# Reordering the attention stage of a retention / MoE kernel: state updates, masks, key scaling and loads

## The reference

```python
gamma = 1.0 - 2.0 ** (-5.0 - np.arange(H, dtype=np.float32))
scale = 1.0 / np.sqrt(D)
state = np.zeros((B, H, D, D), dtype=np.float32)
for t in range(S):
    state = gamma[None, :, None, None] * state + np.einsum('bhd,bhe->bhde', k[:, :, t], v[:, :, t])
    y[:, :, t] = scale * np.einsum('bhd,bhde->bhe', q[:, :, t], state)
```

## Time and profile before

| | us |
|---|---|
| median of 3 runs | 441.89 |
| lowest, highest | 439.13, 443.94 |
| the profiled execution, its own time | 442.01 |
| its span, first to last instruction | 440.3 |
| mean granted TensorE clock | 0.982 of full speed |
| PE busy | 416.1 (95%) |
| DVE, ACT, POOL busy | 211.0 (48%), 196.1 (45%), 154.5 (35%) |

### The profile page before, as it was taken

The page is one execution under the profiler, slowest core; times in us unless marked ns, Lnnn a source line. Parts: engine busy times, 40 slices in busy tenths (PEclk is TensorE's granted clock), DMA queues, the critical chain, the costliest instruction groups (busy, mean ns, idle before and its releaser), DMA issues.

```text
span 440.3 us, 7192 instructions
## 1 busy us (share of the span) xinstructions
PE 416.1 (95%) x2619; PEld 349.8 (79%) x2620; DVE 211.0 (48%) x288; ACT 196.1 (45%) x275; POOL 154.5 (35%) x127
## 2 busy tenths in 40 slices
PE   6699999999999999999659999999999999999992
PEld 3588889897889987878548888888888888888862
DVE  4478838874004878474322612225662261725340
ACT  2234567861214865551612812225771381826440
POOL 3430974000000000025851732213883164563661
PEclk9889999999999999999997999999999999999998
DMA  8979900000420009451573174011288317457100
GB/s 301 416 297 376 423 11 1 0 1 0 155 100 33 1 1 367 205 193 65 222 290 141 49 283 188 30 44 49 69 361 341 118 48 281 151 200 270 35 28 11
DMA packets 15577, 67.75 MB, mean 154 GB/s; under 512 B 2559, under 2 KB 3583, under 8 KB 11200
## 3 DMA queue, kind: packets, MB, share of 16 engines
q1 hardware_dynamic: 12352, 58.88, 34.1%
q0 software_dynamic: 2912, 8.13, 5.6%
q10 hardware_dynamic: 288, 0.41, 0.3%
HBM read 58.49 MB, written 10.22 MB: 156 GB/s over the span
## 4 chain that ended last, share of the span: by engine, by line
PE 86%; DMA 4%; POOL 3%; issue 2%; ACT 1%; SPq 1%; DVE 0%; POOLq 0%; DVEq 0%
PE ps L953 24%; PE ps L955 23%; PE ps L954 23%; PE ps L1240 3%; DMA kv<-qkv 3%; POOL wx L426 3%; PE ps L983 3%; PE ps L1004 2%; PE ps L1001 2%; PE ps L1202 2%; DMA xg<-x_rows,gnow 2%; PE ps L1054 1%; PE ps L967 1%; ACT wx L568 1%; PE ps L1063 1%
## 5 line engine op out<-in xcount | busy, mean ns | idle before, releaser
L426 POOL TENSOR_TENSOR wx<-raw_w,wx 128x1024 fp32r<-128x1024 f32 x21 | 53.5, 2563 | 14.7 <-ACT wx L568 14.6
L953 PE MATMUL ps<-wx,hT 128*128 128x512 f32 x136 | 55.6, 409 | 0.7 <-POOL wx L426 0.7
L568 ACT CAST wx<-raw_w 128x1024 fp32r<-128x1024 f32 x56 | 54.8, 1057 | 1.8 <-issue 1.3
L953 PE MATMUL ps<-wx,xT 128*128 128x512 f32 x136 | 54.6, 402 | 1.0 <-DVE xT L884 0.9
L955 PE MATMUL ps<-wx,hT 128*128 128x512 f32 x136 | 53.8, 396 | 0.0
L954 PE MATMUL ps<-wx,hT 128*128 128x512 f32 x136 | 53.8, 396 | 0.0
L955 PE MATMUL ps<-wx,xT 128*128 128x512 f32 x136 | 53.1, 391 | 0.0
L954 PE MATMUL ps<-wx,xT 128*128 128x512 f32 x136 | 53.0, 390 | 0.0
L628 ACT CAST hT<-ps 128x512 fp32r<-128x512 f32 x34 | 18.3, 591 | 59.5 <-PE ps L1240 59.3
L875 DVE TENSOR_TENSOR wx<-raw_w,wx 128x1024 fp32r<-128x1024 f32 x35 | 42.5, 1262 | 4.6 <-ACT wx L568 3.9
L884 DVE TENSOR_TENSOR xT<-ps,xT 128x512 fp32r<-128x512 f32 x17 | 11.8, 692 | 68.7 <-ACT xT L621 68.7
(11 more groups left out here) (161 smaller groups left out, 809.3 us busy)
## 6 DMA issues: line engine op xcount, KB each, us to landing
raw_w<-w_exp SPq DMA_DIRECT2D x28, 1024.0 KB, 8.0
qk<-qkv SPq DMA_DIRECT2D x7, 768.0 KB, 7.6
kv<-qkv SPq DMA_DIRECT2D x6, 768.0 KB, 9.5
raw_first<-w_exp SPq DMA_DIRECT2D x4, 1024.0 KB, 7.9
x_rows<-x2n SPq DMA_DIRECT2D x12, 256.0 KB, 2.4
x_early<-x2n SPq DMA_DIRECT2D x10, 256.0 KB, 2.1
win_raw<-w_in SPq DMA_DIRECT2D x4, 512.0 KB, 8.9
woutT<-w_out_t SPq DMA_DIRECT2D x1, 2048.0 KB, 13.1
```

Source lines behind the costliest of these rows:

```text
L426: ins = nc.gpsimd.tensor_tensor(wx[:, slot, 1, c], raw, wx[:, slot, 0, c].bitcast(F32), ALU.subtract)
L568: nc.scalar.copy(wx[:, slot, 0, c], raw).then_inc(wx_hi[w], 1)
L953: mm(o, lh, rl, start=first, stop=False)
```

## The change

Four things move, and no arithmetic is added or taken away.
- PE: `updates(i + 1)` stands behind `scores(i + 1, 0)` for every i, not ahead of `values(i, 0)`.
- DVE: `mask(i, 0)` stands ahead of `scan(i)`.
- ACT: `k_scale(i + 2)` stands behind the two copies of pair i.
- SP: `kv` of pairs 2 and 3 comes as keys and values apart (384 KB each), the decay tables of pairs 2 and 3 as 192 KB each behind that pair's values, each with its own semaphore; `updates(i)` waits for the values of pairs 0 to 3, `k_scale` only for the keys.

```diff
--- before.py
+++ after.py
@@ -214,13 +214,14 @@
 
 
         decay0_in = sem("decay0_in")
-        const_in, decay_in, small_in = sem("const_in"), sem("decay_in"), sem("small_in")
+        const_in, small_in = sem("const_in"), sem("small_in")
         first_in, half_in, k0_in = sem("first_in"), sem("half_in"), sem("k0_in")
         loaded = sem("loaded")
         qk_in = [sem(f"qk_in{i}") for i in range(4)]
         kv_in = [sem(f"kv_in{i}") for i in range(4)]
         win_in, wout_in = [sem(f"win_in{n}") for n in range(4)], sem("wout_in")
-        k1_in, decay1_in = sem("k1_in"), sem("decay1_in")
+        k_in = [k0_in] + [sem(f"k_in{i}") for i in range(1, NP_)]
+        decay_in = [decay0_in] + [sem(f"decay_in{p}") for p in range(1, NP_)]
         raw_w1_in = [[sem(f"raw_w1_in{i}{a}") for a in range(2)] for i in range(2)]
         raw_first_in = [[sem(f"raw_first_in{w}{a}") for a in range(2)] for w in range(2)]
         raw_w2_in = [sem(f"raw_w2_in{a}") for a in range(2)]
@@ -324,21 +325,21 @@
             sp.dma_start(kv[0][:, 1, :], qkv[0, :, 3, :]).then_inc(kv_in[0], 16)
             sp.dma_start(decay[:, 0], decay_c[:, 0]).then_inc(decay0_in, 16)
             sp.dma_start(qk[0][:, :, HALF:S], qkv[0, :, 0:2, HALF:S]).then_inc(qk_in[0], 16)
-            sp.dma_start(qk[1][:], qkv[1, :, 0:2, :]).then_inc(qk_in[1], 16)
-            sp.dma_start(kv[1][:, 0, :], qkv[1, :, 2, :]).then_inc(k1_in, 16)
-            sp.dma_start(decay[:, 1], decay_c[:, 1]).then_inc(decay1_in, 16)
-            sp.dma_start(kv[1][:, 1, :], qkv[1, :, 3, :]).then_inc(kv_in[1], 16)
-            for i in range(2, B * NP_):
+            for i in range(1, NP_):
+                sp.dma_start(qk[i][:], qkv[i, :, 0:2, :]).then_inc(qk_in[i], 16)
+                sp.dma_start(kv[i][:, 0, :], qkv[i, :, 2, :]).then_inc(k_in[i], 16)
+                if i == 1:
+                    sp.dma_start(decay[:, i], decay_c[:, i]).then_inc(decay_in[i], 16)
+                sp.dma_start(kv[i][:, 1, :], qkv[i, :, 3, :]).then_inc(kv_in[i], 16)
+                if i > 1:
+                    sp.dma_start(decay[:, i], decay_c[:, i]).then_inc(decay_in[i], 16)
+            for i in range(NP_, B * NP_):
                 j = i % 4
-                if i >= 4:
-                    sp.wait_ge(pv_done, 2 * (i - 4) + 2)
+                sp.wait_ge(pv_done, 2 * (i - 4) + 2)
                 sp.dma_start(qk[j][:], qkv[i, :, 0:2, :]).then_inc(qk_in[j], 16)
-                if i == 2:
-                    sp.dma_start(decay[:, 2:], decay_c[:, 2:]).then_inc(decay_in, 16)
                 sp.dma_start(kv[j][:], qkv[i, :, 2:4, :]).then_inc(kv_in[j], 16)
-                if i >= 4:
-                    c = slice(1024 * (i - 4), 1024 * (i - 4) + 1024)
-                    sp.dma_start(win_raw[:, c], w_in[:, c]).then_inc(win_in[i - 4], 16)
+                c = slice(1024 * (i - 4), 1024 * (i - 4) + 1024)
+                sp.dma_start(win_raw[:, c], w_in[:, c]).then_inc(win_in[i - 4], 16)
                 if i == 5:
                     sp.dma_start(con[:], const_c).then_inc(const_in, 16)
             sp.dma_start(cvw[:], conv_w).then_inc(small_in, 16)
@@ -401,11 +402,8 @@
                 pool.wait_ge(qk_in[j], 16 * (i // 4 + 1))
                 if i == 0:
                     pool.wait_ge(half_in, 16)
-                    pool.wait_ge(decay0_in, 16)
-                if i == 1:
-                    pool.wait_ge(decay1_in, 16)
-                if i == 2:
-                    pool.wait_ge(decay_in, 16)
+                if i < NP_:
+                    pool.wait_ge(decay_in[i], 16)
                 qd = decay[:, p, 2, :].unsqueeze(1).to_broadcast([P, CH, P])
                 nc.gpsimd.tensor_tensor(qs[j][:].rearrange("s (c t) -> s c t", c=CH),
                                         qk[j][:, 0, :].rearrange("s (c t) -> s c t", c=CH), qd,
@@ -523,7 +521,7 @@
 
             def k_scale(i):
                 j, p = i % 4, i % NP_
-                act.wait_ge(k0_in if i == 0 else k1_in if i == 1 else kv_in[j], 16 * (i // 4 + 1))
+                act.wait_ge(k_in[i] if i < 4 else kv_in[j], 16 * (i // 4 + 1))
                 kr = kv[j][:, 0, :].rearrange("s (c h d) -> s c h d", c=CH, h=2)
                 for h in range(2):
                     nc.scalar.activation(kr[:, :, h, :], kr[:, :, h, :], ACT.Copy,
@@ -533,12 +531,12 @@
             k_scale(1)
             for i in range(B * NP_):
                 b, p = i // NP_, i % NP_
-                if i + 2 < B * NP_:
-                    k_scale(i + 2)
                 for g in range(2):
                     n, tb = 2 * i + g, S * b + HALF * g
                     act.wait_ge(pv_done, n + 1)
                     nc.scalar.copy(x1[:, 0, p, tb:tb + HALF], psY[n % 3]).then_inc(yhi_done, 1)
+                if i + 2 < B * NP_:
+                    k_scale(i + 2)
                 for n in {4: (0,), 5: (1, 2), 6: (3,)}.get(i, ()):
                     act.wait_ge(win_in[n], 16)
                     c = slice(1024 * n, 1024 * n + 1024)
@@ -676,7 +674,6 @@
             for p in range(NP_):
                 gc = con0[:, C_GC + (CH - 1) * p:C_GC + (CH - 1) * (p + 1)].unsqueeze(1).to_broadcast([P, D, CH - 1])
                 nc.vector.tensor_copy(gpow[:, p, :].rearrange("d (e c) -> d e c", e=D), gc).then_inc(made, 1)
-            dve.wait_ge(decay0_in, 16)
             dve.wait_ge(made, 8)
             dve.wait_ge(zeroed, 2)
 
@@ -693,10 +690,8 @@
 
             def mask(i, g):
                 p, n = i % NP_, 2 * i + g
-                if i == 1 and g == 0:
-                    dve.wait_ge(decay1_in, 16)
-                if i == 2 and g == 0:
-                    dve.wait_ge(decay_in, 16)
+                if i < NP_ and g == 0:
+                    dve.wait_ge(decay_in[i], 16)
                 dve.wait_ge(s_done, n + 1)
                 if n >= 2:
                     dve.wait_ge(pv_done, n - 1)
@@ -715,8 +710,8 @@
             scan(0)
             mask(0, 1)
             for i in range(1, B * NP_):
+                mask(i, 0)
                 scan(i)
-                mask(i, 0)
                 y_lo(i - 1, 0)
                 mask(i, 1)
                 y_lo(i - 1, 1)
@@ -959,7 +954,7 @@
                 pe.wait_ge(k_scaled, 2 * i + 2)
                 if i:
                     pe.wait_ge(st_done, 2 * i)
-                if i < 2:
+                if i < 4:
                     pe.wait_ge(kv_in[i], 16)
                 for c in range(CH - 1):
                     for h in range(2):
@@ -1012,13 +1007,10 @@
             warm_up(2, psY[2])
             pe.wait_ge(zeroed, 2)
             for i in range(B * NP_):
-                if 0 < i and i + 1 < B * NP_:
-                    updates(i + 1)
                 values(i, 0)
                 if i + 1 < B * NP_:
                     scores(i + 1, 0)
-                if i == 0:
-                    updates(1)
+                    updates(i + 1)
                 values(i, 1)
                 if i + 1 < B * NP_:
                     scores(i + 1, 1)
```

## The result

| | before | changed |
|---|---|---|
| median of 9 runs, us | 440.81 (439.13 to 443.94) | 436.64 (434.6 to 437.8) |
| profiled execution, its own time and span | 442.01, 440.3 | 436.53, 434.8 |
| attention stage ends (gate matmuls begin) | 55.59 | 51.17 |
| mean granted TensorE clock | 0.982 | 0.992 |

The ratio is 0.9902 (95% interval 0.9874 to 0.993): about 1% faster. By the time alone two rivals fit equally well, 0.8 us to either side: the stream of loads at full rate (437.4) and PE alone (435.9). Of the 2.6 us, 1.2 are the starting point: the forecast counts from the 442.0 of the profiled execution, and the median of nine is 440.81. Counted by the medians the gain is 4.2 us, where 2.8 was forecast.

The account below looks back on a forecast made before the run. Bound: PE's early wait for pair 2's kv, then PE alone, with the load-to-POOL chain level in the tail. With that chain setting pair 7's q at 50.1, the stage ends 2.8 us earlier: 442.0 - 2.8 = 439.2, range 436.0 to 442.4.

Parts of the forecast that it names:

- the stream of loads at full rate: Rival: loads up to pair 7's kv come at 416 GB/s, not the slow 376; time 437.4, chance 0.15.
- PE alone: Rival: the chain over POOL does not hold PE in the attention stage, whole 6.1 us comes; 435.9, chance 0.12.
- The gap at 16 and its clock: PE's 3.89 us wait for pair 2's kv shrinks by 3.7 us; no clock fall there saves 2.4 us.
- The stretched supply: Pair 2's scaled keys at 17.0, values later, decay near 18.0 and q at 19.8, ahead of PE's need at 21.2.
- The steady period: PE's time per pair in the attention stage stays 5.12 us; DVE's scan has 0.6 us of cover; booked 0.
- The second bound over POOL: In pairs 6 and 7, q follows kv's landing by 6.5 us; PE waits 2.4 us before pair 6's values.
- The landing of the loads: kv of later pairs lands 2.0 us earlier (bounds 1.5 and 2.8): pair 6 at 37.9, pair 7 at 43.6.
- bound (a): Least gain of the load stream: pair 5's qk, back to back at 376 GB/s, lands at 29.5, earlier by 1.5.
- rival 1: Loads up to pair 7's kv come at 416 GB/s; stage ends at 50.95, time 437.4, chance 0.15.
- The low clock in the new wait: Rivals: clock falls in PE's wait before pair 6's values, mildly (440.3, chance 0.14) or fully (442.0, chance 0.14).
- the mild form: Rival: clock low half as long as before in PE's wait before pair 6's values; costs 1.1, time 440.3, chance 0.14.
- The rule on batches: Skill's advice to batch DMAs to at least 1 MiB; by it the cut loads take 0.9 us longer, giving 440.1.

Follow-up runs that it names:

- e3: Kernel before with 24 filler matmuls on zeros on PE ahead of pair 2's update; ratio to before 0.998 (0.995 to 1.001), median 439.02 us.
- e5: Kernel before with POOL's q multiplies moved ahead of its low parts of w_in; ratio to before 1.001 (0.999 to 1.003), median 440.60 us.
- e12: Changed kernel with POOL's q ahead of its low parts and DVE's old order back (scan ahead of mask); ratio to before 0.996, median 439.21 us.
- e8: Changed kernel with POOL's q ahead of its low parts and PE's old order back (update ahead of values); ratio to before 1.000, median 440.15 us.
- e4: Changed kernel with POOL's q multiplies ahead of its low parts of w_in; ratio to before 0.986 (0.983 to 0.989), median 432.95 us.
- e7: Changed kernel with SP holding pair 5's loads back by one pair, so the DMA queue runs dry; ratio to before 0.997, median 439.38 us.
- e2: Kernel before with the new PE, DVE and ACT orders but the old loads; ratio to before 0.996 (0.993 to 1.000), median 437.12 us.
- e9: Changed kernel unaltered, run and traced a second time; ratio to before 0.992 (0.990 to 0.993), median 437.26 us.

## Why the prediction was right or wrong, point by point

- **The gap at 16 and its clock: right for the execution it was read from.** PE's wait went, the clock stayed; against that execution e3 shows the clock's share as 2.3 us (priced 2.4), but e5's trace has 1.4 and e3's times 0.8 (-0.6 to 2.2). The stretched supply was in time as worked out, with the decay of pair 2 landing at 18.3 to 18.4 (forecast 18.0).
- **The steady period: right.** 5.11 us in the changed kernel. It holds only with all three orders: with DVE's back the mask lengthens it to 5.79 (e12), with PE's back the wait for ACT's key scaling to 5.90 (e8).
- **The second bound over POOL: right.** The wait before pair 6's values was 1.99 us (forecast 2.4), ended by POOL's q; q came 6.3 us behind `kv` (forecast 6.5), and e4 removes the wait by POOL's order alone, which does nothing on the kernel before (e5).
- **The landing of the loads: mis-sized.** This is the term that was off: "I take 2.0, nearer to the first". `kv` of pair 6 landed at 36.92 rather than 39.90, that of pair 7 at 42.02 rather than 45.65: 3.0 and 3.6 earlier, both outside my bounds of 1.5 and 2.8. The two streams are level up to the first `w_in` quarter, which landed at 27.5 (27.4 before). Closing the gap brought what bound (a) says: pair 5's `qk` landed at 29.4 (worked out 29.5), its `kv` at 31.4 rather than 32.9. The other 1.5 and 2.1 us are the rate behind it. I held the 376 GB/s of 33 to 44 us in the kernel before, which is 335 to 383 between 34 and 42, to be the rate of this stretch of the program, but with a queue that never ran dry it was 393 to 447 GB/s between 24 and 46. That was rival 1's case, to which I gave 0.15. With it the sum has the stage end at 50.95, measured 51.17.
- **Where luck came in.** The time is inside the range although both landings lie outside their bounds: the range was drawn wide for the rivals. With the starting point of 442.0, 1.2 us above the median, the gain was forecast as 2.8 us and is 4.2 by the medians.
- **The low clock in the new wait: a mixture, not a case.** I gave it 0.28 as if one execution stood for all. Of the two traces of the changed kernel one has it, at a price of 1.5 us (forecast 1.1 for the mild form, after 0.6 of slack before q of pair 7; that slack was not there, since q and PE were level).
- **The rule on batches:** by the Trainium skill, "DMA: Bandwidth & Descriptors", section Bandwidth, the cut loads would have been slower; the prediction's estimate by it was some 0.9 us (1.0 by its own figures). The stretches of 2 us from 12 to 24 have a mean of 406 GB/s with the cut loads and 414 without, some 0.2 us of the 12, and the first `w_in` quarter behind them lands 0.1 us later. The trace does not agree with the rule for loads queued one behind the other.
- **The sign and the 1%:** I gave 0.26 to more than 1% faster. The ratio is 0.990, on the border itself.

What stays open: why a queue that has run dry moves less for some stretches later (below), how often the clock falls in a wait of 2 us, and how the gain is shared between loads and orders, since stage ends and times give different shares.

## What to carry to other kernels

A prefetch that waits for a consumer's progress turns an early stall into a late one: here a gap of 3.9 us on PE left the DMA queue empty 9 us later and loads landing late 25 us later. So price such a gap by what is issued behind it as well, and ask where the gain ends: the changed kernel was held by work of low urgency (casts for the next stage) that stood ahead of urgent work in another engine's queue, and moving it was worth another 1.9 us. And try the orders of a hand-written schedule in sets: here PE's order undone alone cost 5.5 to 5.8 us of the stage, all three undone 1.8 to 2.1. Last, a price read from one execution is that execution's: hold a second trace of the unchanged kernel beside it.

## What the runs showed of the hardware that was not expected

- **A dry DMA queue and slow stretches.** The four traces in which the queue ran dry near 24 to 28 (before, e3, e5, e7) all have later stretches of 2 us at 290 to 383 GB/s (335 to 383 at 34 to 42; 290 and 355 at 30 to 34; 340 and 376 at 38 to 42; 362 and 328 at 30 to 34; in e3 the queue was short of work only from 25.5 to 26.5), with the DMA share at 0.9 or more. The ten in which it did not have none below 393 between 24 and 46. The two go together in all 14 traces, and in e7 one moved wait brought both; that is one trace of the direct test, and the mechanism is open.
- **The clock and short waits.** PE's waits of 1.99 and 2.16 us (changed kernel, e2) left the clock at 2.4 GHz; waits of 2.10 and 2.09 us (e9, e7) were followed by a fall to 1.2. The first wait for the gather, near 211 to 217 us, says the same: it is 2.30 to 2.68 us long in 13 traces, and the clock falls in or behind it in six (2.34 to 2.68) and not in the other seven (2.30 to 2.67). The length of the wait alone doesn't decide it.
